# Decayed linear attention and a mixture of experts on one core: the next chunk's scores in two parts, the first load and the first mask product in halves, a new order in the head, two products of the tail placed later

## The reference

```python
for t in range(S):
    state = gamma[None, :, None, None] * state + np.einsum('bhd,bhe->bhde', k[:, :, t], v[:, :, t])
    y[:, :, t] = scale * np.einsum('bhd,bhde->bhe', q[:, :, t], state)
...
for b in range(B):
    prev_e = -1
    for s in range(S):
        fresh_e = int(np.argmax(logits[b, s]))
        if s == 0 or local_gate[b, s] < 0.5:
            e = fresh_e
        else:
            e = prev_e if prev_e >= 0 else fresh_e
        prev_e = e
        ls = logits[b, s] - logits[b, s].max()
        p = np.exp(ls)
        p /= p.sum() + 1e-09
        h = np.maximum(x[b, s] @ w1[e], 0.0)
        out[b, s] = p[e] * (h @ w2[e])
```

## Time and profile before

| What | us |
|---|---|
| median of 3 runs | 258.63 |
| the profiled execution, its own time | 259.11 |
| span of the profiled execution | 257.4 |
| TensorE busy | 245.7 |
| VectorE busy | 190.8 |
| ScalarE busy | 133.6 |
| GpSimd busy | 65.0 |

### The profile page before, as it was taken

The page is one execution under the profiler, slowest core; times in us unless marked ns, Lnnn a source line. Parts: engine busy times, 40 slices in busy tenths (PEclk is TensorE's granted clock), DMA queues, the critical chain, the costliest instruction groups (busy, mean ns, idle before and its releaser), DMA issues.

```text
span 257.4 us, 5058 instructions
## 1 busy us (share of the span) xinstructions
PE 245.7 (95%) x1932; PEld 211.4 (82%) x1932; DVE 190.8 (74%) x414; ACT 133.6 (52%) x254; POOL 65.0 (25%) x57
## 2 busy tenths in 40 slices
PE   6999989999999999999999999999999999999991
PEld 2787877887887988988988898898899889889891
DVE  3352988897996895999799688768859868886700
ACT  1223537546659373467438557545834844754310
POOL 0473145661004332005301500510330051011011
PEclk9999999999999999999999999999999999999999
DMA  5999999972201937356808936762791884440000
GB/s 169 368 414 410 415 410 411 388 311 83 84 1 41 362 104 258 149 216 229 353 1 327 359 125 244 281 281 51 318 397 40 306 311 187 171 194 13 0 38 13
DMA packets 11387, 56.83 MB, mean 221 GB/s; under 512 B 1751, under 2 KB 2135, under 8 KB 9570
## 3 DMA queue, kind: packets, MB, share of 16 engines
q1 hardware_dynamic: 7056, 45.96, 46.0%
q0 software_dynamic: 2560, 7.34, 8.1%
q10 hardware_dynamic: 1746, 3.19, 3.3%
HBM read 50.20 MB, written 7.34 MB: 224 GB/s over the span
## 4 chain that ended last, share of the span: by engine, by line
PE 80%; DMA 6%; DVE 5%; ACT 5%; issue 2%; POOLq 0%; SPq 0%; ACTq 0%; DVEq 0%
PE ps L1298 18%; PE ps L1317 10%; PE ps L1319 10%; PE ps L1318 10%; PE ps L1300 9%; PE ps L1170 5%; PE ps L1219 5%; DMA x_gathered<-x_rows,gather_idx 4%; PE ps L1230 4%; PE ps L1278 3%; PE ps L1341 2%; ACT slot_values L553 2%; PE ps L1189 2%; DMA qkv_sb<-qkv 2%; PE ps L1203 1%
## 5 line engine op out<-in xcount | busy, mean ns | idle before, releaser
L1298 PE MATMUL ps<-x_sorted_T,w_split 128*128 128x240 f32 (+6 forms) x288 | 84.5, 362 | 0.1
L1300 PE MATMUL ps<-x_sorted_T,w_split 128*128 128x120 f32 (+6 forms) x288 | 72.7, 252 | 0.0
L853 DVE TENSOR_TENSOR w_split<-w_raw,w_split 128x1024 fp32r<-128x1024 f32 x56 | 66.1, 1220 | 7.5 <-ACT w_split L559 7.5
L559 ACT CAST w_split<-w_raw 128x1024 fp32r<-128x1024 f32 x56 | 55.8, 1041 | 5.7 <-DMA w_raw<-w 5.7
L1298 PEld LDWEIGHTS ps<-x_sorted_T,w_split 128*128 128x128 f32 x288 | 54.2, 188 | 4.2 <-issue 0.7
L1300 PEld LDWEIGHTS ps<-x_sorted_T,w_split 128*128 128x128 f32 x288 | 54.9, 191 | 0.3
L867 DVE TENSOR_REDUCE h_sums<-ps 128x120 f32<-128x240 f32 (+6 forms) x72 | 40.3, 561 | 19.6 <-PE ps L1300 18.8
L569 ACT ACTIVATE hT<-h_sums 128x120 fp32r<-128x120 f32 (+6 forms) x72 | 26.0, 365 | 51.5 <-DVE h_sums L867 51.3
L1317 PE MATMUL ps<-w_split,hT 128*128 128x512 f32 x120 | 48.3, 402 | 0.0
L1319 PE MATMUL ps<-w_split,hT 128*128 128x512 f32 x120 | 47.4, 395 | 0.0
L1318 PE MATMUL ps<-w_split,hT 128*128 128x512 f32 x120 | 47.4, 395 | 0.0
(11 more groups left out here) (146 smaller groups left out, 259.0 us busy)
## 6 DMA issues: line engine op xcount, KB each, us to landing
w_raw<-w SPq DMA_DIRECT2D x14, 2048.0 KB, 9.4
qkv_sb<-qkv SPq DMA_DIRECT2D x22, 512.0 KB, 12.4
w_raw<-w SPq DMA_DIRECT2D x8, 512.0 KB, 15.1
x_rows<-x_rows_sb ACTq DMA_DIRECT2D x12, 256.0 KB, 6.3
qkv_sb<-qkv SPq DMA_DIRECT2D x2, 256.0 KB, 13.3
x_gathered<-x_rows,ident_and_w_router POOLq DMA_INDIRECT x12, 8.4
out<-y_rows,ident_and_w_router POOLq DMA_INDIRECT x12, 5.1
c_route_sb<-c_route SPq DMA_DIRECT2D x1, 152.0 KB, 9.5
```

The costliest lines, as they stand in the source:

```text
L559: nc.scalar.copy(ws[:, par, 0, half, at:at + PIECE], raw[:, half, at:at + PIECE]).then_inc(w_hi_rdy[half], 1)
L853: V.tensor_tensor(ws[:, par, 1, half, at:at + PIECE], raw[:, half, at:at + PIECE], ws[:, par, 0, half, at:at + PIECE].bitcast(fp32), ALU.s ...
L1298: MM(at[:, 0:2 * w].rearrange("p (a t) -> p a t", a=2), ws[:, par, 0, 0, cols], xTs[:, k, :, sub], start=(k == 0), stop=(k == KD - 1), ski ...
L1300: last = MM(at[:, w:2 * w], ws[:, par, 1, 0, cols], xTs[:, k, 0, sub], start=False, stop=(k == KD - 1), skip_group_check=True)
```

## The change

- The first transfer, queries and keys of chunk 0, becomes two transfers of 256 KB, one for head pairs 0 and 1 and one for 2 and 3, with a semaphore each; `qk(0)` waits for the second between its halves.
- The first mask product becomes two, and `from_chunk(0)` waits for the second one between its halves.
- The first run of `keep_warm` has 9 products for 10.
- `qk(1)` stands ahead of `state_products(0)`.
- From chunk 2 on `qk(m+1)` is cut: 3 head pairs ahead of `rows_and_logits(m-1)`, the fourth behind it and behind the small routing products `to_col` and the table's first product. In chunk 5 it is two and two.
- `up(0, 7)` stands ahead of `first_unit`.
- Of `down(0, f, 1)` the blocks 0 and 1 stand ahead of the two `x_transpose` of the second unit.

```diff
@@ SP @@
-            load_half(0, 0)
+            for half, done in enumerate((qk_in[0], qk_first)):
+                at = slice(half * HP // 2, (half + 1) * HP // 2)
+                sp.dma_start(io[:, 0, 0:2, at, :], qkv[0:P, 0:2 * DM].rearrange(
+                    "p (a n t) -> p a n t", a=2, n=HP)[:, :, at, :]).then_inc(done, 16)
             load_half(0, 1)
@@ DVE, masked(m) @@
+                if m == 0:
+                    for half, done in enumerate((m_ready, first_masked)):
+                        at = slice(half * HP // 2, (half + 1) * HP // 2)
+                        V.tensor_tensor(sm[:, 0, :, at, :], bank(0, 2).rearrange("p (r n t) -> p r n t", r=2, n=HP)[:, :, at, :],
+                                        masks[:, :, at, :], ALU.mult).then_inc(done, 1)
+                    return
@@ PE @@
-            def qk(m):
+            def qk(m, heads=range(HP)):
...
-                pe.wait_ge(qk_in[s], 16 * (m // SLOTS + 1))
-                if m > 0:
-                    pe.wait_ge(m_ready, m)
-                for n in range(HP):
+                if heads[0] == 0:
+                    pe.wait_ge(qk_in[s], 16 * (m // SLOTS + 1))
+                    if m > 0:
+                        pe.wait_ge(m_ready, m)
+                for n in heads:
+                    if m == 0 and n == HP // 2:
+                        pe.wait_ge(qk_first, 16)
...
-                last.then_inc(qk_done, 1)
+                if heads[-1] == HP - 1:
+                    last.then_inc(qk_done, 1)
@@ from_chunk @@
                 for n in heads:
+                    if m == 0 and n == 2:
+                        pe.wait_ge(first_masked, 1)
@@ head @@
-            keep_warm(10, 7)
+            keep_warm(9, 7)
...
             from_chunk(0)
+            qk(1)
             state_products(0)
-            qk(1)
...
             for m in range(2, NX):
+                ahead = HP // 2 if m == NC - 1 else HP - 1
                 if m + 1 < NX:
-                    qk(m + 1)
+                    qk(m + 1, range(0, ahead))
...
+                if m + 1 < NX:
+                    qk(m + 1, range(ahead, HP))
                 if m % NC < NC - 1:
                     state_products(m)
@@ tail of the routing @@
             up(0, 6, 0, 0, ROWS)
+            up(0, 7, 0, 0, ROWS)
             first_unit()
-            up(0, 7, 0, 0, ROWS)
...
+            pe.wait_ge(dm, 1)
+            for f in range(2):
+                down(0, f, 1, 0)
             for s in range(2):
                 x_transpose(1, s)
-            pe.wait_ge(dm, 1)
-            for f in range(KF):
+            for f in range(2, KF):
                 down(0, f, 1, 0)
```

More of the change, by code:

```diff
@@ L267, in bass_retention_moe_kernel @@
         masking = sem("mask_product_begun")
+        first_masked = sem("second_half_of_first_masked_ready")
+        qk_first = sem("second_half_of_first_qk_in")
         s_ready = sem("state_ready")
```

## The result

The changed kernel takes 260.79 us (median of 11 runs, 259.31 to 261.40) against 259.47 for the kernel before in the same comparison (258.46 to 260.22); the ratio is 1.0054, with an interval of 1.0032 to 1.0077. It is slower by half a per cent, where the forecast was 0.4% faster, and 260.79 lies outside the range. The profiled execution took 260.23 us, with a span of 258.3.

What follows compares the result with a forecast made beforehand. TensorE, busy 95% of the span with 11.7 us idle, was taken as the bound. Head -0.60, loop -0.20, `first_unit` +0.30 and transposes -0.49 sum to -0.99 us: 257.6 us against 258.63, 0.4% faster, range 256.4 to 258.9.

Steps and rivals of the forecast that it cites:

- Cutting the scores in two costs no pass: Loop: splitting the scores adds no TensorE time, each head pair 0.27 us; the whole loop gives -0.20 us.
- the price at `rank`: Loop, chunks 5 and 8: the later mask product delays `route_c` and so `rank`, +0.41 and +0.20 us.
- Chunks 7 and 10: ScalarE's nine `slot_values` set the pace, 0: Loop, chunks 7 and 10: ScalarE's slot values set the pace, so the cut changes nothing, 0 us.
- rival C: Ahead of `rank`, chunks 5 and 8: GpSimd's `k_decayed` holds VectorE, 2.1 us lost, 259.8 us in all; chance 0.10.
- the first step of `route_c` is not held: Ahead of `rank`: this VectorE step reads one input from the accumulator, so GpSimd does not hold it.
- The loop's mechanism: Row-copy waits go in chunks 2, 5, 6 and 9; a wait of 0.5 to 0.8 us precedes chunk 5's `rank`.
- The head, -0.60: Start of the kernel: halved first load and mask, one filler fewer, earlier `qk(1)` give 0.60 us, ends 0.90 and 0.40.
- The 6.36: Head: the time in us at which the first load's whole 512 KB were taken to be there.
- the later loads: Head: every load after the first comes 0.3 us later, making `state_products(1)` wait for `k_decayed(1)`.
- Rival B: Head: the halved load gives nothing, second half at 7.0, -0.39 us remains, 258.2 us; chance 0.26.
- `first_unit`, +0.30: End of the routing: `first_unit` behind `up(0, 7)` starts 0.30 us later and delays the second unit's gather as much.
- The transposes, -0.49: Second unit: six products of `down` cover the gather, so TensorE's wait before the transposes goes, -0.49 us.
- The cover of 0.35 us: Third unit: transposed rows and weight splits are ready 0.35 us before the next `up`; otherwise 0.5 us is given back.

Runs made afterwards that it cites:

- experiment 1: Changed kernel with the next chunk's scores whole again, head and tail still changed: 258.41 us against 259.11 for the kernel before, ratio 0.9979.
- experiment 2: Kernel before with only the scores cut in two around the rows: 261.25 us against 259.11, ratio 1.0070.
- experiment 6: Changed kernel with the split-off score passes placed directly ahead of `from_state`: 266.12 us against 258.95 for the kernel before, ratio 1.0252.
- experiment 10: Kernel before with one tiny product ahead of the last four score passes, 128 rows in chunk 4, 64 in chunk 5: 258.75 us against 259.53.
- experiment 3: Changed kernel with `prob_low` ahead of `slot_col_match` on VectorE: 260.01 us against 259.11 for the kernel before, ratio 1.0033.
- experiment 8: Kernel before with only `first_unit` moved behind `up(0, 7)`: one run, 258.83 us against 258.95.
- experiment 7: Kernel before with only the second unit's transposes behind six products of `down(0, ., 1)`: 258.51 us against 258.95, ratio 1.0001.
- experiment 4: Changed kernel without the cut and with `first_unit` ahead of `up(0, 7)` again: 259.03 us against 259.11 for the kernel before, ratio 0.9995.
- experiment 9: Kernel of experiment 4 with scores cut only in chunks 2, 3 and 4, each in another proportion: one run, 261.14 us against 259.53 for the kernel before.
- experiment 5: Kernel before with only the new head (halved first load and mask, one filler fewer, earlier `qk(1)`): 258.74 us against 258.95, ratio 0.9983.

## Why the prediction was wrong

- **"Cutting the scores in two costs no pass"** is the first step that failed. I worked in starts and gave a head pair a quarter of a whole group, 0.27 us. But a group is 0.21 + 4 x 0.22 = 1.09: it has a price that does not shrink with it, and a cut pays it twice. Experiments 1 and 2 show that the cut alone makes the loop 2.0 us longer, and 6 and 10 that the price needs neither the rows nor a wait. What inside TensorE makes the price no run shows. It is 0.21 us in a chunk, and 0.44 in chunk 5, which is cut 8 and 8. Chunks 3 and 4 show it bare, +0.20 for 0. In chunks 2, 6 and 9 it leaves 0.11 to 0.16 of the 0.32 us, in starts, that each wait was. In chunk 8 it lies on top of the price at `rank`: +0.42 for +0.20.
- **"Chunks 7 and 10: ScalarE's nine `slot_values` set the pace, 0"** is the second. That ScalarE sets the pace was right, and it hides most of the cut's own price there (5.60 us in experiment 3 against 5.52); but I did not ask what ScalarE waits for. It is VectorE's `prob_low`, queued behind the mask product, and this had 0.24 us of room before GpSimd's `q_decayed`. The cut in chunk 6 takes 0.29 of it. The loss of 0.93 us is all in this (experiment 3: 0.85 come back by the order alone).
- So **rival C's** mechanism came, in another place than where I had looked for it: I had asked which instruction stands beside `k_decayed` in chunks 5 and 8, and the one that was held stands beside `q_decayed` in chunk 7. It had 0.10 with me. That the first step of `route_c` is not held was right (0.17 us in both kernels). The rule of the Trainium skill (SBUF — State Buffer, section "Who interferes with whom"), that VectorE with two SBUF inputs and GpSimd reading SBUF exclude each other for a whole instruction, is borne out by this trace too: `prob_low` reads two such inputs and took 1.23 us for 0.15. I had used the rule to clear one instruction, and not to list those it applies to.
- **The loop's mechanism was else as forecast**: the four waits for the copy of the rows, in chunks 2, 5, 6 and 9, went, and waits ahead of `rank` came in chunks 5 and 8 (0.80 and 0.32 us).
- **The head, -0.60**: the pair of profiles gives -0.61, by luck. The 6.36 on which I built was one execution's: in old heads the first scores start at 5.66 and 5.73 too (experiments 8 and 7). Like with like it is -0.22, and over all profiles -0.06. The halves did their part, as no new head in nine profiles waits for the first load; the filler did not, and the later loads, which I had put at 0.3 us and at `k_decayed(1)`, come first at `from_chunk(0)` or `qk(1)` (1.01 us above). `k_decayed(1)` is waited for in experiment 4 too, 0.37 us. Rival B's head, which stands still, was nearer in size than the forecast, but not in its cause: it had the second half land at 7.0, and here all 16 passes had run by 6.42.
- **`first_unit`, +0.30**: right at its own place (+0.28), +0.20 at the third unit.
- **The transposes, -0.49**: a wait read from one execution, mis-sized as a gain of every execution. Neither of the two other profiles in which nothing else of the tail or the clock was touched (experiments 2 and 10) has it, and the timed runs of experiment 7 show no gain. The cover of 0.35 us that I had called thin held.

With the sizes measured the sum is +1.99 in the loop, about -0.1 for the head, and between -0.5 and +0.2 for the tail, +1.4 to +2.1; timed were +1.3, with an interval of 0.8 to 2.0.

## What to carry to other kernels

A group of short products on TensorE has a price for starting and stopping that a mean per product hides; before cutting one, look for the same instruction in groups of two sizes, and if the profile has none, take the price as unknown and positive. Where a moved step delays an instruction, follow it on the other engines until something waits for nothing: here 0.3 us at a mask product became 0.9 us of TensorE's time at an instruction of three elements, because GpSimd got there first. And a wait for a transfer, or for the clock, in a single profile is one draw; what is worth a change is a wait that a second profile shows too.

## What I had not expected of the hardware

- Score passes over 64 rows cost 0.21 us more when a product over 128 rows stands among them, and 0.10 when one over 64 rows does (experiment 10). The first 8 of 16 passes take 0.76 us where they stand first and 0.65 behind (experiment 9); this is not explained.
- The same 10 or 9 fillers leave TensorE at the lower rate until 4 to 6 us in some executions and until 10 us in others, with the granted clock shown as 1.00 in both; this moves the scores of chunk 3 by 1.1 to 1.6 us.
- In the profile of experiment 5 the granted clock was 0.72 on average from 76 to 82 us, at the end of the routing, and 0.50, the lower of its two levels, from 78.0 to 81.3. The tail took 35.42 us, 1.2 more than the 34.2 of an old tail at full clock. Experiment 9's profile has the same fall and a tail of 35.43. Both had waited 0.47 us ahead of `first_unit` before it, but so did profiles without a fall (0.46); what sets it off is open. In experiment 6 the fall came behind the wait of 2.70 us (window of experiment 5, its length, TensorE's busy time and count, the granted clock, the share of the DMA engines, GB/s):

```profile
76.00:82.00 6.00, 5.53 (x26) 0.72 0.17 44
```
